# When GpSimd adds up the next dense weight, and when VectorE normalises the last head: an attention + two-MoE kernel on one Trainium2 core

## What is computed

```
attn = exp(masked scores); attn /= sum(attn) + 1e-09; x = attn @ v      # 16 heads, 768 x 64 each
P = exp(x @ w_gate - max)
for _ in range(8):                     # Sinkhorn
    P /= P.sum(1) + 1e-09              # rows: over the 8 experts
    P /= P.sum(0) + 1e-09; P *= N / E  # columns: over the 1536 tokens
for e in range(8):                     # dense: every token through every expert
    out += P[:, e] * (relu(x @ w1[e]) @ w2[e])
```

## Time and profile before

| | us |
|---|---|
| time, median of 3 runs | 1404.18 (1402.83 to 1405.65) |
| time of the profiled execution | 1407.4 |
| its span, first to last instruction | 1405.6 |
| PE busy in the span | 1330.7 (95%) |
| DVE busy | 884.1 (63%) |
| ACT busy | 583.1 (41%) |
| POOL busy | 298.5 (21%) |

### The profile page before, as it was taken

How to read it: one execution, slowest core, us unless ns; L and a number is a source line. 1 busy time by engine, 2 the same in 40 slices (tenths; PEclk the granted TensorE clock), 3 DMA queues, 4 the chain that set the end, 5 groups by cost and what they waited for, 6 DMA issues and landing times.

```text
span 1405.6 us, 25010 instructions
## 1 busy us (share of the span) xinstructions
PE 1330.7 (95%) x9507; PEld 762.3 (54%) x9507; DVE 884.1 (63%) x1555; ACT 583.1 (41%) x909; POOL 298.5 (21%) x210
## 2 busy tenths in 40 slices
PE   6999999789999999999999999999999999999996
PEld 3666666555446545545644654554464455556664
DVE  5999999777657525723742753573374366567993
ACT  6999999753104303411420440232143043226671
POOL 5765666230200300300200030030011000021221
PEclk9999999999999999999999999999999999999998
DMA  8334331123102001101100200110110023467940
GB/s 225 80 97 101 78 78 39 61 74 123 61 26 94 1 1 60 60 0 60 60 0 14 82 23 0 60 60 0 60 60 0 0 77 116 154 212 269 340 147 19
DMA packets 49567, 107.87 MB, mean 77 GB/s; under 512 B 4600, under 2 KB 6776, under 8 KB 49504
## 3 DMA queue, kind: packets, MB, share of 16 engines
q1 hardware_dynamic: 47264, 103.63, 23.0%
q0 software_dynamic: 2240, 3.35, 0.6%
HBM read 93.63 MB, written 17.34 MB: 79 GB/s over the span
## 4 chain that ended last, share of the span: by engine, by line
PE 76%; DVE 11%; issue 6%; ACT 3%; POOL 2%; DMA 1%; SPq 0%; ACTq 0%; DVEq 0%; POOLq 0%
PE ps L1561 14%; PE ps L1562 14%; PE ps L1563 14%; PE ps L1585 8%; PE ps L1588 8%; PE ps L1587 8%; PE ps L1483 2%; DVE probsT_lo L958 2%; DVE row_max L964 2%; ACT probsT_hi L707 1%; PE ps L1493 1%; DVE x_lo L1036 1%; PE ps L1471 1%; PE ps L1473 1%; DVE h L1234 1%
## 5 line engine op out<-in xcount | busy, mean ns | idle before, releaser
L1585 PE MATMUL ps<-x_hi,w_hi 128*128 128x384 f16 x896 | 293.5, 328 | 13.9 <-ACT x1s L793 5.8
L1561 PE MATMUL ps<-w_hi,h 128*128 128x512 f16 x768 | 291.8, 380 | 2.3 <-DVE w_lo L1074 2.3
L1587 PE MATMUL ps<-x_lo,w_hi 128*128 128x384 f16 x896 | 293.7, 328 | 0.0
L1588 PE MATMUL ps<-x_hi,w_lo 128*128 128x384 f16 x896 | 293.5, 328 | 0.0
L1563 PE MATMUL ps<-w_hi,h 128*128 128x512 f16 x768 | 291.7, 380 | 0.0
L1562 PE MATMUL ps<-w_lo,h 128*128 128x512 f16 x768 | 291.6, 380 | 0.0
L1194 DVE SCALAR_TENSOR_TENSOR x<-ps,gate_now,x 128x512 f32<-128x512 f32 x84 | 63.1, 751 | 264.3 <-PE ps L1563 264.0
L793 ACT ACTIVATE x1s<-ps 128x384 f32<-128x384 f32 x64 | 30.4, 475 | 370.4 <-PE ps L1588 370.4
L571 POOL TENSOR_TENSOR wf<-wf 128x1024 f32<-128x1024 f32 x8 | 22.1, 2758 | 635.1 <-DMA wf<-w1a 635.1
L814 ACT ACTIVATE h<-parts 128x1152 f16<-128x1152 f32 x64 | 74.4, 1162 | 153.6 <-DVE parts L1152 153.6
L1585 PEld LDWEIGHTS ps<-x_hi,w_hi 128*128 128x128 f16 x896 | 88.0, 98 | 77.1 <-ACT x1s L793 8.1
(11 more groups left out here) (219 smaller groups left out, 2338.0 us busy)
## 6 DMA issues: line engine op xcount, KB each, us to landing
wf<-w1a SPq DMA_DIRECT2D x32, 512.0 KB, 5.8
w_stage_in<-w2a SPq DMA_DIRECT2D x8, 2048.0 KB, 8.8
w_in<-w1b SPq DMA_DIRECT2D x4, 2048.0 KB, 9.3
w_in<-w2b SPq DMA_DIRECT2D x4, 2048.0 KB, 9.9
w_in_b<-w1b SPq DMA_DIRECT2D x4, 2048.0 KB, 10.2
w_in_b<-w2b SPq DMA_DIRECT2D x4, 2048.0 KB, 10.1
rows<-blank SPq DMA_DIRECT2D x1, 6682.0 KB, 21.1
qk_in<-qT SPq DMA_DIRECT2D x32, 192.0 KB, 4.0
```

The costliest lines, as they stand in the source:

```text
L1561: pe.matmul(acc, a_hi, b_hi, start=(m == 0), stop=False)
L1585: pe.matmul(group_bank(g, role), w_hi, x_hi, start=(opens and kt == 0), stop=False, skip_group_check=not opens)
L1587: pe.matmul(group_bank(g, role), w_hi, x_lo, start=False, stop=False, skip_group_check=not opens)
L1588: last = pe.matmul(group_bank(g, role), w_lo, x_hi, start=False, stop=(kt == 1), skip_group_check=not opens)
```

## The change

Three edits:

- GpSimd's loop over experts now begins at expert 2 and waits for `mm1_done >= 56 e` first: the sums of expert e's w1 come after the last block product of expert e-1. For expert 1 the four sums stand ahead of the loop, and each waits for one more `columns_in`.
- ACT's `w1_part` waits for the load, and for the sums only from combination 3 on (0 to 2 are blocks as they were loaded).
- At the seam DVE's `x7_lo_part(0, 0)` is moved from before `sum_up` to behind `sum_x(0)`.

```diff
-            def sum_w1(e):
+            def sum_w1(e, turn=lambda n: None):
 
                 pool.wait_ge(w1_loaded, 64 * e + 64)
+                turn(0)
                 pool.tensor_tensor(wf[:, 5, :, :], wf[:, 0, :, :], wf[:, 3, :, :], ALU.subtract
                                    ).then_inc(w1_summed, 1)
+                turn(1)
...
-            with pool.Fori(1, E) as e:
+            sum_w1(1, lambda n: pool.wait_ge(columns_in, n + 1))
+            with pool.Fori(2, E) as e:
+                pool.wait_ge(mm1_done, NM1 * e)
                 sum_w1(e)
...
             def w1_part(e, k):
                 act.wait_ge(mm1_done, NM1 * e)
-                act.wait_ge(w1_summed, 4 * e + 4)
+                act.wait_ge(w1_loaded, 64 * e + 64)
+                if k >= 3:
+                    act.wait_ge(w1_summed, 4 * e + 4)
...
-            x7_lo_part(0, 0)
-
             sum_up(G - 1, 0)
             sum_up(G - 1, 1)
             normalise(G // 2 - 1, 1)
 
             sum_x(0)
-            for k in range(1, 4):
+            for k in range(4):
                 x7_lo_part(0, k)
```

More of the change, by code:

```diff
@@ L566, in _ @@
             split_v(1, 1, 0)
-            def sum_w1(e):
+            def sum_w1(e, turn=lambda n: None):
                 pool.wait_ge(w1_loaded, 64 * e + 64)
+                turn(0)
                 pool.tensor_tensor(wf[:, 5, :, :], wf[:, 0, :, :], wf[:, 3, :, :], ALU.subtract
                                    ).then_inc(w1_summed, 1)
+                turn(1)
                 pool.tensor_tensor(wf[:, 3, :, :], wf[:, 3, :, :], wf[:, 2, :, :], ALU.add).then_inc(w1_summed, 1)
+                turn(2)
                 pool.wait_ge(w1_summed, 4 * e + 2)
@@ L576, in sum_w1 @@
                                    ).then_inc(w1_summed, 1)
+                turn(3)
                 pool.wait_ge(w1_summed, 4 * e + 3)
```

## The result

| | before | changed |
|---|---|---|
| time, median | 1402.83 (1401.04 to 1405.65, 5 runs) | 1391.62 (1389.62 to 1394.72, 5 runs) |
| profiled execution | 1407.4 | 1389.6 |
| its span | 1405.6 | 1387.8 |
| PE busy | 1330.7 | 1325.0 |
| DVE busy | 884.1 | 877.2 |

The changed kernel takes 0.992 of the time before, 95% interval 0.9901 to 0.9939: 11.2 us off, where 12.6 were forecast, and its time of 1391.62 us stands beside the forecast 1391.5. (The forecast was counted from a median of three runs, 1404.18 us; the five runs here have 1402.83.)

The account below looks back on a forecast made before the run. PE was taken to bound the kernel, with time won only where it stands still or runs slowly. 6.8 + 4.75 + 1.05 = 12.6 us off the median 1404.18 gave 1391.5 us, range 1388 to 1396.8.

Parts of the forecast that it names:

- Edit 1: Experts 2 to 7, first product: sums moved out remove PE's wait for x1s, six times 1.14, 6.8 us.
- the rival of the group's own rhythm: First products, experts 2 to 7: the 1.14 us come from group rhythm, not sums; 1398.3 us, chance 0.04.
- the best count: Second product: VectorE's split isn't held by GpSimd's sums; 4 us of cover before PE needs the update of x.
- the worst: Second product: split waits for second sum, copy for third, to T+8.6 (T: PE's last block product); 1.0 us cover.
- Edit 2: Expert 1's sums in the Sinkhorn stage: spacing them saves 2.95 us of wait and 1.80 of slow clock, 4.75 us.
- Price zero for the spaced sums: Sinkhorn stage: steps late by some tenths with 2 us to spare each; price zero, bound 0 to 0.6 us.
- the clock's share of it (1.80): Sinkhorn stage: PE ran eight to ten matmuls at the lower clock after its wait, 1.80 us more than 5.31.
- Edit 3: Seam: normalising the last head first moves PE's wait and brings later operations forward; gain 1.05 us.
- another order than I took: Seam: one VectorE sum (0.95), GpSimd's L607 (1.80), VectorE's other sum, taking turns, end at about 275.1.
- the clock rival: Seam: PE's clock falls after the second wait too and the 1.05 us don't come; 1394.4 us, chance 0.12.
- no window past 290 would be below full clock: Sign against the forecast: a granted clock below 1 in a dense window past 290 us would prove it wrong.
- The slower rival: Second product: sums starve VectorE, PE waits 1.6 us at tile 2 of six experts; 1401.1 us, chance 0.03.

Follow-up runs that it names:

- only_late: Kernel before plus only the wait for mm1_done in GpSimd's loop, for all experts from 1 on: 1398.22 us, ratio 0.9945.
- act_waits: Changed kernel with ACT waiting for all four sums again for experts 2 to 7: 1393.97 us, ratio 0.9911.
- only_spaced: Kernel before plus only expert 1's sums spaced one per Sinkhorn step and ACT's shorter wait: 1400.94 us, ratio 0.9969.
- only_seam: Kernel before plus only the seam edit, the last head normalised first: 1405.97 us, ratio 0.9997.
- six_sums: Changed kernel with the first sum done three times for experts 2 to 7, six sums instead of four: 1393.19 us, ratio 0.9907.
- before_six: Kernel before with the first sum done three times for experts 1 to 7, six sums instead of four: 1409.55 us in one run.
- lo_first: Changed kernel with gate operations later, expert 0's w2 parts earlier, and GpSimd's later low halves of x's second half waiting for VectorE's: 1385.79 us, ratio 0.986.
- changed_again: The changed kernel itself, measured again on another chip's runs beside lo_first: 1392.71 us, ratio 0.9916.

## Why the prediction held, point by point

**Edit 1: 6.8 forecast, 6.86 in the traces.** Expert 1 to expert 7 took 707.42 us and takes 700.56. only_late shows that it is the place of the sums; act_waits, that ACT's earlier start has no part in experts 2 to 7; the rival of the group's own rhythm falls with the wait's being gone. In the new place the split waited for nothing, as on the best count; the copy stood nearly a whole sum, as on the worst, but it was the second sum and not the third, so it ended at T + 6.2 and not T + 8.6.

**Edit 2: 4.75 forecast, 68.00 - 63.26 = 4.74 in the traces.** Price zero for the spaced sums was right: no pair came late. That the clock's share of it (1.80) can come or not from one execution to the next was not in my count: some kernels with a clean chain show 64.8 to 64.9, one slow stretch behind another wait. only_spaced gives 4.6 in medians.

**Edit 3: 1.05 forecast, 1.33 at the place it was forecast, and nothing to be seen in the time.** The steps came in another order than I took (VectorE's second sum was held, 2.44 us, and GpSimd's first, 2.55), and ended at 274.65 where I had 275.1. PE resumed 19.57 us after A before, and 18.24 in the change. The step that failed is the last: that PE, ahead at 285, is still ahead 65 us later. It is what the clock rival said: in only_seam at the very place, behind the second wait, and in the changed kernel in others. There, behind the first seam wait, PE ran slowly for longer: the granted clock of 273 to 282 us was 0.81 before and 0.62 in the change, which PE's shorter wait at 285.27 (1.30 in place of 2.71) hid. Then, windows of the changed kernel:

```profile
332.00:334.00 2.00, 2.00 (x36) 1.33 (x33) 0.03 (x1) 0.18 (x1) 0.00 (x0) 0.75 0.00 0
334.00:336.00 2.00, 2.00 (x7) 0.91 (x6) 0.00 (x0) 0.49 (x1) 0.00 (x0) 0.50 0.00 0
```

The kernel before is at full clock there, but has its slow stretch earlier and longer, in part under waits of PE for `x_lo`, where it costs nothing:

```profile
318.00:320.00 2.00, 1.76 (x7) 0.58 (x6) 2.00 (x2) 0.23 (x1) 1.01 (x1) 0.50 1.06 375
```

At the second product 0.60 of the 1.33 are left in this execution, and only_seam is 0.7 behind the kernel before; its ten timed runs show no gain. That no window past 290 would be below full clock was wrong as a test, for the kernel before has such windows itself, which I had not read. What exactly sets these stretches stays open.

**The sum.** 12.6 us forecast, 12.41 in the traces up to expert 7, of which 0.21 is the attention stage; 11.2 between the medians (0.9901 to 0.9939 of the time, 8.6 to 13.9 us). The sum is sound within that interval; that 1391.5 and 1391.62 agree to 0.1 us is luck. From the median of the five runs, 1402.83, the same sum gives 1390.2, and edit 3's 1.05 us, which is in it, can't be found in the times. The slower rival, VectorE starved in the second product, falls with six_sums.

## What to carry to other kernels

When one engine holds up another by reading the same memory, ask of each held operation who waits for it. Moving the same work to a place where nobody waits gave 7 us here, and half as much work again in that place cost nothing to be seen. A gain measured at one place of the timeline is only a gain if the next waits and clock stretches leave it standing: try each part alone, with enough runs. And read where the kernel before is slow already, ahead of naming a slow stretch as the sign of an error.

## What the runs showed of the hardware that I had not expected

PE's clock fell not only behind waits. In the changed kernel it went to half pace at 333 us right behind some 120 matmuls of 16 columns, in which PE had no idle time at all:

```profile
332.56 0.17 PE L1580 MATMUL ps<-gates,x_lo 128*128 128x16 f16 x1
...
333.14 0.53 PE L1591 MATMUL ps<-x_hi,w_hi 128*128 128x384 f16 x1
```

A matmul of 384 columns took 0.53 us there in place of 0.33. The kernel before, with the same 120 matmuls, kept its clock. The clock fell at that place in four other traces of the 13 (before_six, six_sums, act_waits, lo_first) and not in the other eight, changed_again among them. A wait was no surer sign: of the 17 waits of 2.3 to 2.8 us from 284 to 372 us, 9 had a slow stretch at or just behind their end. The wait of 2.3 us before the second product had one in four traces of ten, that of 2.71 us had none, that of 2.57 in only_seam and that of 2.78 had one. Where a stretch came there and nothing else held PE up, the stage took 64.8 to 64.9 us in place of 63.26: 1.5 to 1.7 us. The Trainium skill (TensorE: Matmul & The Clock Gate, Part 1) has half rate as the state after idling and full rate after sustained work; the row at 333.14 differs from it, since there was no idling right ahead, and the measurement decides.
